# Front of a fused attention and two-MLP kernel: column norms by TensorE, softmax in two halves, split score steps, a new order of the first unit

## What is computed

```
qn = q / (norm(q, axis=tokens) + 1e-6)      # one norm per channel (column)
kn = k / (norm(k, axis=tokens) + 1e-6)
s  = kn.T @ qn / tau                        # 256 x 256
a  = exp(s - max_row(s)); a /= sum_row(a) + 1e-9
x  = v @ a                                  # read as N x 256
x  = gelu(x @ w_in1) @ w_out1               # h * sigmoid(1.702 h)
y  = elu(x @ w_in2) @ w_out2
```

## Time and profile before

| | |
|---|---|
| time, median of 3 runs | 1051.01 us (1050.25 to 1051.07) |
| time of the profiled execution | 1050.98 us |
| its span | 1049.2 us (1.8 us lie around it) |
| PE busy, DVE, ACT, POOL | 98%, 73%, 72%, 1% |
| mean granted PE clock | 0.996 |
| front part, span start to the first `down` product | 72.94 us |

### The profile page before, as it was taken

How to read it: one execution, slowest core, us unless ns; L and a number is a source line. 1 busy time by engine, 2 the same in 40 slices (tenths; PEclk the granted TensorE clock), 3 DMA queues, 4 the chain that set the end, 5 groups by cost and what they waited for, 6 DMA issues and landing times.

```text
span 1049.2 us, 13911 instructions
## 1 busy us (share of the span) xinstructions
PE 1032.1 (98%) x4588; PEld 860.5 (82%) x4588; DVE 763.2 (73%) x1236; ACT 758.0 (72%) x1358; POOL 10.1 (1%) x11
## 2 busy tenths in 40 slices
PE   9999999999999999999998999999999999999996
PEld 7878888888888888888986887887887888888896
DVE  6688756656656655655878788888888888788775
ACT  6586665665666566556778888788788788788884
POOL 0110000000000000000000000000000000000000
PEclk9999999999999999999999999999999999999998
DMA  9913003003003002003122002101201101110112
GB/s 351 285 36 61 1 23 59 1 7 74 1 1 76 3 0 58 1 1 121 41 78 79 1 1 61 21 1 41 40 1 41 33 9 35 22 21 1 21 21 35
DMA packets 106935, 46.24 MB, mean 44 GB/s; under 512 B 90864, under 2 KB 97776, under 8 KB 106224
## 3 DMA queue, kind: packets, MB, share of 16 engines
q1 hardware_dynamic: 106864, 45.36, 16.0%
HBM read 33.03 MB, written 12.32 MB: 43 GB/s over the span
## 4 chain that ended last, share of the span: by engine, by line
PE 91%; ACT 4%; issue 2%; DVE 1%; DMA 0%; DVEq 0%; ACTq 0%; SPq 0%
PE bank L932 29%; PE bank L934 29%; PE bank L933 29%; PE bank L944 4%; ACT xo L599 1%; ACT act_out L537 1%; ACT blk_hi L461 1%; DVE gated L772 1%; PE bank L998 0%; PE bank L999 0%; PE bank L1003 0%; DMA qk<-in_k_dram 0%; ACT g_hi L555 0%; ACT u L497 0%; ACT w_dn_hi L423 0%
## 5 line engine op out<-in xcount | busy, mean ns | idle before, releaser
L932 PE MATMUL bank<-g_hi,w_dn_hi 128*128 128x512 f32 (+1 forms) x768 | 296.3, 386 | 0.7 <-DVE g_lo L785 0.6
L934 PE MATMUL bank<-g_hi,w_dn_lo 128*128 128x512 f32 (+1 forms) x768 | 295.9, 385 | 0.0
L933 PE MATMUL bank<-g_lo,w_dn_hi 128*128 128x512 f32 (+1 forms) x768 | 295.8, 385 | 0.0
L785 DVE TENSOR_TENSOR g_lo<-gated,g_hi 128x512 fp32r<-128x512 f32 (+1 forms) x384 | 259.9, 677 | 48.5 <-ACT g_hi L555 42.4
L932 PE MATMUL bank<-blk_hi,w_up_hi 128*128 128x512 f32 (+1 forms) x672 | 261.5, 389 | 4.1 <-DVE gated L772 1.6
L933 PE MATMUL bank<-blk_lo,w_up_hi 128*128 128x512 f32 (+1 forms) x672 | 259.0, 385 | 0.0
L934 PE MATMUL bank<-blk_hi,w_up_lo 128*128 128x512 f32 (+1 forms) x672 | 259.0, 385 | 0.0
L555 ACT CAST g_hi<-gated 128x512 fp32r<-128x512 f32 (+1 forms) x288 | 175.8, 610 | 21.8 <-DVE gated L772 21.8
L932 PEld LDWEIGHTS bank<-g_hi,w_dn_hi 128*128 128x128 f32 x768 | 144.2, 188 | 28.8 <-DVE g_lo L785 1.8
L933 PEld LDWEIGHTS bank<-g_lo,w_dn_hi 128*128 128x128 f32 x768 | 144.2, 188 | 27.0
L934 PEld LDWEIGHTS bank<-g_hi,w_dn_lo 128*128 128x128 f32 x768 | 144.2, 188 | 27.0
(11 more groups left out here) (110 smaller groups left out, 718.1 us busy)
## 6 DMA issues: line engine op xcount, KB each, us to landing
qk<-in_q_dram SPq DMA_DIRECT2D x14, 384.0 KB, 9.9
qk<-in_k_dram SPq DMA_DIRECT2D x14, 384.0 KB, 10.7
x_scratch<-xo SPq DMA_DIRECT2D x10, 512.0 KB, 3.1
raw<-x_scratch SPq DMA_DIRECT2D x5, 1024.0 KB, 4.8
out_dram<-blocks SPq DMA_DIRECT2D x40, 128.0 KB, 2.7
blocks<-in_v_dram SPq DMA_DIRECT2D x36, 128.0 KB, 3.4
stage<-in_moe_w_in_dram SPq DMA_DIRECT2D x8, 512.0 KB, 5.9
stage<-in_moe_w_out_dram SPq DMA_DIRECT2D x8, 512.0 KB, 5.4
```

The costliest lines, as they stand in the source:

```text
L785: nc.vector.tensor_tensor(g[1][:, x, 0:w], gated[:, n % 2, 0:w], g[0][:, x, 0:w].bitcast(F32), ALU.subtract).then_inc(c_glo, 1)
L932: nc.tensor.matmul(out_ps, w_hi, x_hi, start=start, stop=False, skip_group_check=goes_on)
L933: nc.tensor.matmul(out_ps, w_hi, x_lo, start=False, stop=False, skip_group_check=goes_on)
L934: return nc.tensor.matmul(out_ps, w_lo, x_hi, start=False, stop=stop, skip_group_check=goes_on)
```

## The change

- **Groups.** 20 groups now: 2, 1, 1, 2, twelve of 3, then 2, 1, 1, 1. The first 17 (`LANES`) go through the lanes.
- **Idle turns.** The three dummy matmuls become 14 fp32 matmuls of 128 columns on `ones`, which POOL writes first.
- **Split steps.** In groups 5 to 15 one step each, and groups 17 and 18, is scored by three fp32r passes per half instead of one fp32 matmul. ACT makes the high part (`split_hi`), POOL the low one, DVE for the last two.
- **Norms.** The fold on DVE is gone. The squares of the last three groups go to SBUF, ACT copies the three lanes to SBUF, and PE sums each of these six tiles by four fp32 matmuls with one moving column (`column_sums`), ahead of the last step of group 16. q's and k's norms are then four columns; q's is turned into a row by two fp32 matmuls on the identity (`norm_row`).
- **Halves.** The scores of groups 17 to 19 are done for half 0 first, then for half 1, and the softmax, its transposes and `eT` run by halves between the v transposes.
- **Order.** SP issues v between the parts 1 and 2 of w_in1. ACT splits w_in1 after the norms; the lists of ACT, DVE and PE up to unit 1 are new. The number of `a_w`, product and transpose instructions is the same.

```diff
-    G_STEPS = [3] * 14 + [2, 1, 1, 1]
-    LANES = 15
+    G_STEPS = [2, 1, 1, 2] + [3] * 12 + [2, 1, 1, 1]
+    LANES = NG - 3
+    SPLIT_GROUPS = list(range(5, 16)) + [LANES, LANES + 1]
+    BY_GPSIMD = 11
+    PARTS = 7
+    SQUARES_UP_TO = list(range(1, 15)) + [15, 18, NG, NG, NG, NG]
...
-        aw_ps = banks[4:8]
+        aw_ps = banks[6:8] + banks[4:6]
-        q_sums, k_sums = banks[4][:, 0:C], banks[2][:, 0:KC]
-        eT_ps = banks[2]
+        col_sums, row_ps = banks[4][:, 0:2 * KC], banks[4][:, C:2 * C]
+        eT_ps = [banks[i][:, 0:C] for i in (2, 4)]
...
+        IDLE_TURNS = 14
...
-            for fb in range(FB):
-                load_w_in1(fb)
+            load_w_in1(0)
+            load_w_in1(1)
...
+            load_w_in1(2)
+            load_w_in1(3)
...
+            for i, n in enumerate(SPLIT_GROUPS[:BY_GPSIMD]):
+                pool.wait_ge(c_qkhi, i + 1)
+                nc.gpsimd.tensor_tensor(qk_lo[:, i % PARTS, :, :], qk[:, n % RING, :, 0, :],
+                                        qk_hi[:, i % PARTS, :, :].bitcast(F32), ALU.subtract).then_inc(c_qklo, 1)
...
+            def split_hi(n):
+                i = SPLIT_GROUPS.index(n)
+                act.wait_ge(c_qk[n % RING], 32 * (n // RING + 1))
+                if i >= PARTS:
+                    act.wait_ge(c_score, SPLIT_GROUPS[i - PARTS] + 1)
+                nc.scalar.copy(qk_hi[:, i % PARTS, :, :], qk[:, n % RING, :, 0, :]).then_inc(c_qkhi, 1)
...
+            squared = 0
+                if n == LANES:
+                    act.wait_ge(c_sum, SUM_ZERO + LANES)
+                    nc.scalar.copy(lanes[:, :, :, :], sums[:, :, :, :]).then_inc(c_lanes, 1)
+                if n in SPLIT_GROUPS:
+                    split_hi(n)
+                while squared < SQUARES_UP_TO[n]:
+                    square(squared)
+                    squared += 1
...
+            act.wait_ge(c_norm, 1)
+            nc.scalar.activation(roots, col_sums, ACT.Sqrt).then_inc(c_root, 1)
+            nc.scalar.activation(small[:, 1:2], small[:, 1:2], ACT.Exp)
             w1_hi(0)
-            act.wait_ge(c_norm, 1)
+            w1_hi(1)
...
+            def et_hi(i):
+                act.wait_ge(c_et, i + 1)
+                nc.scalar.copy(eT[0][:, :, i * P:(i + 1) * P], eT_ps[i].rearrange("p (j i) -> p j i", j=KC)).then_inc(c_ethi, 1)
...
+            et_hi(0)
+            w1_hi(2)
+            sum_of_row()
+            et_hi(1)
             nc.scalar.activation(small[:, 1:2], small[:, 1:2], ACT.Gelu_apprx_sigmoid)
+            aw_raw(0)
             block_hi(0, X11)
             block_hi(0, X21)
-            aw_raw(0)
             aw_raw(1)
+            w1_hi(3)
+            up_hi(0, 0)
             block_hi(0, T2)
-            up_hi(0, 0)
             up_hi(0, 1)
-            dn_hi(0)
             block_hi(0, T1)
             aw_raw(2)
+            up_hi(0, 2)
+            copy_u1(0)
+            aw_raw(3)
+            dn_hi(0)
             block_hi(0, T3)
+            up_hi(1, 0)
+            up_hi(1, 1)
+            copy_u2(0)
+            gelu(0, H11)
             block_hi(0, T4)
-            up_hi(0, 2)
-            aw_raw(3)
-            copy_u1(0)
-            up_hi(1, 0)
+            g_hi(0, H11)
+            copy_u3(0)
             aw_raw(4)
             block_hi(0, X22)
-            copy_u2(0)
             aw_raw(5)
-            gelu(0, H11)
-            copy_u3(0)
-            g_hi(0, H11)
             aw_raw(6)
-            up_hi(1, 1)
             gelu(0, H22)
             aw_raw(7)
             g_hi(0, H22)
...
+            dve.wait_ge(c_root, 1)
+            step(nc.vector.tensor_scalar_add(roots, roots, 1e-6))
+            step(nc.vector.reciprocal(inv_q, inv_q))
+            assert steps_done[0] == N_INV_Q
+            step(nc.vector.tensor_scalar(inv_k, inv_k, tau_sb, None, ALU.mult))
+            step(nc.vector.reciprocal(inv_k, inv_k))
-            dve.wait_ge(c_score, NG)
+            dve.wait_ge(c_norm, 2)
+            nc.vector.tensor_copy(rq_row[:], row_ps).then_inc(c_row, 1)
+            dve.wait_ge(c_row, 1)
             for i in range(KC):
+                dve.wait_ge(c_half, i + 1)
...
+            et_lo(0)
+            inverse_of_row()
             copy_v(0)
-            dve.wait_ge(c_rsum, 1)
-            step(nc.vector.reciprocal(inv_sum, row_sum))
-            dve.wait_ge(c_ethi, 1)
-            nc.vector.tensor_tensor(eT[1][:, :, :].rearrange("p j i -> p (j i)"), eT_ps[:],
-                                    eT[0][:, :, :].rearrange("p j i -> p (j i)").bitcast(F32),
-                                    ALU.subtract).then_inc(c_etlo, 1)
+            et_lo(1)
             t_of(0, T1)
             copy_v(1)
             t_of(0, T2)
-            t_of(0, T3)
             block_lo(0, X11)
             block_lo(0, X21)
+            up_sums(0)
+            up_lo(0, 0)
             block_lo(0, T2)
-            up_lo(0, 0)
-            up_sums(0)
-            t_of(0, T4)
-            dn_lo(0, 0)
+            block_lo(0, T1)
+            t_of(0, T3)
             up_lo(0, 1)
-            block_lo(0, T1)
             up_lo(0, 2)
             sum11_of(0)
+            t_of(0, T4)
             block_lo(0, T3)
+            dn_lo(0, 0)
+            up_lo(1, 0)
             up_sums(1)
             block_lo(0, T4)
-            block_lo(0, X22)
             sum22_of(0)
             g_lo(0, H11)
+            block_lo(0, X22)
+            up_lo(1, 1)
             dn_lo(0, 1)
-            up_lo(1, 0)
-            up_lo(1, 1)
...
-            pe.wait_ge(c_zero, 1)
-            for turn in range(3):
-                nc.tensor.matmul(s_ps[turn % KC], scores[:, 0, 0:P], scores[:, 0, :], start=turn < KC, stop=False)
+            pe.wait_ge(c_const, 1)
+            for _ in range(IDLE_TURNS):
+                nc.tensor.matmul(s_ps[0][:, 0:P], ones[:], ones[:], start=True, stop=True)
...
+            def split_step(n, i):
+                part = SPLIT_GROUPS.index(n)
+                if part < BY_GPSIMD:
+                    pe.wait_ge(c_qklo, part + 1)
+                else:
+                    pe.wait_ge(c_qklast, part - BY_GPSIMD + 1)
+                hi, lo, rows = qk_hi[:, part % PARTS, :, :], qk_lo[:, part % PARTS, :, :], slice(i * P, (i + 1) * P)
+                return three_pass(s_ps[i], hi[:, 1, rows], lo[:, 1, rows], hi[:, 0, :], lo[:, 0, :], False, False, True)
+            def column_sums(of, start, stop):
+                for x in range(2 * KC):
+                    mm = nc.tensor.matmul(col_sums[:, x:x + 1], of[:, x // KC, (x % KC) * P:(x % KC + 1) * P], ones[:, 0:1],
+                                          start=start and x == 0, stop=stop, skip_group_check=True)
+                return mm
             def norms():
-                pe.wait_ge(c_fold, GROUP + NG - LANES)
+                for x in range(NG - LANES):
+                    pe.wait_ge(c_sq, LANES + x + 1)
+                    column_sums(sq_last[x], x == 0, False)
+                pe.wait_ge(c_lanes, 1)
+                for lane in range(GROUP):
+                    mm = column_sums(lanes[:, lane, :, :], False, lane == GROUP - 1)
+                mm.then_inc(c_norm, 1)
+            def norm_row():
+                pe.wait_ge(c_dve, N_INV_Q)
+                    mm = nc.tensor.matmul(row_ps[:, i * P:(i + 1) * P], inv_q[:, i:i + 1].to_broadcast([P, P]), ident[:],
...
+            for n in range(LANES):
+                pe.wait_ge(c_qk[n % RING], 32 * (n // RING + 1))
+                split = 1 if n in SPLIT_GROUPS else 0
+                for s in range(split, G_STEPS[n]):
+                    if n == LANES - 1 and s == G_STEPS[n] - 1:
+                        norms()
+                    for i in range(KC):
+                        mm = whole_step(n, s, i)
+                if split:
+                    for i in range(KC):
+                        mm = split_step(n, i)
+                mm.then_inc(c_score, 1)
+            norm_row()
+            for n in range(LANES, NG):
+                pe.wait_ge(c_qk[n % RING], 32 * (n // RING + 1))
+            for i in range(KC):
+                for n in range(LANES, NG):
+                    mm = split_step(n, i) if n in SPLIT_GROUPS else whole_step(n, 0, i)
+                mm.then_inc(c_half, 1)
...
+                if d == 0:
+                    pe.wait_ge(c_vfirst[tile], V_LOAD)
...
+                if n < KC:
+                    pe.wait_ge(c_ethi, i + 1)
+                if n == 2:
+                    pe.wait_ge(c_etlo, KC)
+                if n == 3:
                     pe.wait_ge(c_vcopy, KC)
                 if n >= 4:
+                if n < KC:
+                    pe.wait_ge(c_etlo, i + 1)
...
-            for n in range(5):
-                a_w(n)
+            transpose_first(0)
+            transpose_exp(0)
+            transpose_first(1)
+            transpose_exp(1)
+            transpose_first(2)
+            a_w(0)
+            transpose_first(3)
+            a_w(1)
+            a_w(2)
+            a_w(3)
```

(43 more changed lines are left out.)

113 lines of the change are left out of this document (39 added, 74 removed).

## The result

The changed kernel is slower: median 1056.71 us (1056.41 to 1057.17, 5 runs) against 1051.01 us for the kernel before on the same chip, a ratio of 1.0054 (1.0039 to 1.0069). That is outside the range of the prediction (1047.7 to 1053.0). The profiled execution took 1056.41 us, 5.43 more than that of before.

What follows compares the result with a forecast made beforehand. PE, busy 98% of the span, was taken as the bound, with only its time up to the first `down` product movable. -1.05 - 1.85 + 5.05 - 3.35 = -1.2 us gave 1049.8 us, range 1047.7 to 1053.

Steps and rivals of the forecast that it cites:

- Term 1: The start: turns on `ones` raise PE's clock, so scores start at 6.3 at full clock; -1.05 us, or -1.45.
- rival (d): At the start: the dummies don't raise the clock before the scores do; +1.0 to +1.8 us, 1051; chance 0.1.
- Data is no limit: At the start: three-step groups land every 1.96 to 2.0 us, while PE needs 2.59 for one.
- Term 2: The 13 split steps: 26 fp32 matmuls become 78 passes of 256 columns at 0.12 us; -1.85 us.
- Rival (b): In the split steps: passes of 256 columns wait for their weights; at 0.188 us each, 1055.1; chance 0.08.
- Term 3: The norms: 48 one-column records at 0.112 us and four of `norm_row` added on PE, 0.79 us removed; +5.05 us.
- Rival (a): Behind the norms: the clock falls to half for 3.4 us, moving the end by 1.65; 1051.4; chance 0.2.
- term 4: Softmax to the first `down` product: idle time and slow clock of 4.85 us become 1.5 idle; -3.35 us.

Runs made afterwards that it cites:

- e11: The kernel before with only the 14 turns on `ones` in place of its three dummies, without the memset of `scores`: 1050.18 us, ratio 0.9990 to before.
- e3: The changed kernel with the edits of e1 and e2 together: 1055.46 us, ratio 1.0052 to before.
- e10: e7 with POOL making all 13 low parts, w_in1 loaded and split in another order, two of the last squares in PSUM: 1047.82 us, ratio 0.9963 to before.
- e5: The changed kernel without POOL's 11 split steps, which are scored whole; DVE's two stay split: 1059.26 us, ratio 1.0081 to before.
- e1: The changed kernel with all four high parts of w_in1 made ahead of ACT's root: 1055.07 us, ratio 1.0040 to before.
- e2: The changed kernel with 128 moving columns of `ones` in the norm matmuls in place of one: 1054.01 us, ratio 1.0032 to before.
- e6: e2 with the last low part of w_in1 made by DVE behind `w_up_lo` instead of by POOL: 1051.28 us, ratio 1.0007 to before.
- e7: The changed kernel with last squares and lanes folded on DVE into one tile, 8 one-column records instead of 48: 1050.22 us, ratio 0.9994 to before.
- e8: e7 with w_in1's parts 0 and 1 split ahead of the root, one part later, one last: 1053.28 us, ratio 1.0022 to before.
- e9: e7 with all four parts of w_in1 loaded ahead of v and split ahead of the root: 1052.10 us, ratio 1.0010 to before.

## Why the prediction was wrong, step by step

| step | predicted | in the kernel after |
|---|---|---|
| scores start | 6.3, full clock | 6.02, full clock |
| norms start | 41.9 | 41.68 |
| norms end | 47.3 | 48.13 |
| from there to the first `a_w` | 5.9 | 8.06 |
| first `a_w` to the first `down` | 18.5 | 22.46 |
| first `down` | 71.7 | 78.65 |

**Term 1 was right, its size in part by luck.** The turns bring the clock up ahead of the scores, and rival (d) falls; in e11 the turns alone bring the norms 1.43 us earlier, the better of my two values (1.05 and 1.45). But with the same turns the scores start anywhere from 5.67 to 7.05 in the eleven traces, and my 6.3 is one value out of that. "Data is no limit" holds only just: PE waits for a landing 0.20 us at 11.70 in e3 (scores from 6.04) and 0.37 at 9.71 in e10 (from 5.72).

**Term 2 was right, its price by a small cancelling.** Passes follow at 0.12 as forecast (15.82 to 15.94 to 16.05 in a step); the first pass behind a plain fp32 matmul takes 0.31, but the eight fp32 records behind the step take 1.54 us (16.41 to 17.95) where eight at 0.216 take 1.73, so 0.19 comes back. e5 confirms 0.13 us saved per step. Rival (b), loads that don't overlap, falls. The lower of the two prices that I weighed, from the Trainium skill's "TensorE: Matmul & The Clock Gate", section "Back-to-back issue gap" (262 cycles), isn't what these rows show: 0.12, not 0.109.

**Term 3 was right in the row's price and wrong as a term.** A record costs 0.108 to 0.112, as forecast, while the clock is up. 1.07 us more (6.45 for 5.38) came from the clock's fall within the norms; in e1, where it fell only at their end, the same 48 records take 5.33. (Two small sums are off: term 3 adds up to +5.03, not +5.05, and the idle and slow part of the old stretch to 4.80, not 4.85. Neither matters.)

**Rival (a) came, with a price too small.** I gave it 0.2 and 1.65 us, from the one fall in the trace of before, 3.4 us long. It lasted 6.82 us. In it lie 24 norm records (+1.27 by 3.86 - 2.59), and from 48.13 to 52.49 PE gets 4.36 us of half speed, 2.2 us of work lost; that is the 8.06 - 5.9. Together 3.4 us. The evidence "L954 was only 0.36 us long, so no row tests this" should have weighed for a high chance, not a low one: the one argument against it, that short transposes left the clock up, was about another kind of instruction and 1.2 us of it. The Trainium skill, "TensorE: Matmul & The Clock Gate", "Part 4: PE-mode transpose", says that transposes don't count as busy. No run here tests that. What e2 shows beside the kernel after is that one-column matmuls let the clock fall, and that 128 columns in the same place are enough to keep it.

**Two steps failed.** The first is the full clock that terms 3 and 4 take for granted through the norms and behind them, which I had only as rival (a) at 1.65 us: it cost 1.07 + 2.16 = 3.2. The second, and larger, is the walk of term 4, which lays out DVE's operations with their old durations and so puts what DVE loses beside POOL at nothing. It reads "POOL's low parts of w_in1 come at 5.3, 7.7, 10.0, 13.9 ...: no wait". I used POOL's lateness as POOL's only effect, and I had the sentence "POOL did 1024 columns in 2.34 us with DVE busy beside it" for the converse, which it doesn't hold: it gives POOL's duration, and says nothing about what DVE lost. The old list hid it, because POOL worked from 49.93 to 56.94, where DVE mostly read PSUM. The trace of before did show it once, in a row that I read past. DVE in the kernel before:

```profile
55.93 1.56 DVE L734 TENSOR_TENSOR t_sum<-raw,t_sum 128x512 f32<-128x512 f32 x1
57.42 0.68 DVE L734 TENSOR_TENSOR t_sum<-raw 128x512 f32<-128x512 f32 x1
```

Two operations of one line and size, 1.56 and 0.68, the long one ending 0.55 us behind POOL's 56.94. The new order put the last low part at 61.73, amid DVE's chain to `product1`, and PE stood idle for 2.5 us; with the 1.7 of the second fall of the clock, less 0.24 for the rest, this makes the +3.96 from `a_w` to `down`. e6 takes POOL away from there, and the wait goes from 2.67 to 0.48, so some 2.2 us of it are the meeting. That the second fall comes from the wait is likely, not shown: it came behind waits of 2.35 (the kernel after), 2.33 (e5) and 2.60 (e7), not behind one of 2.67 (e2) or 1.87 (e8), and in e1, e3, e6, e9 and e10, with no wait over 0.5 us ahead of `product1`, it didn't come. The Trainium skill, "GPSIMD Engine Reference", section "8. Key points", states that GpSimd shares its SBUF interfaces with VectorE, with contention for instructions in a two-port mode or with two SBUF inputs. The trace agrees for the two inputs (2.62 beside 0.42). That section gives no price, and the price is what decided. Had I laid it into the walk, the stall would have been in the sum.

The difference is thus, from 71.7: -0.2 (start and splits), +1.07 (norms), +2.16 (half clock behind them), +3.96 = 78.7, against 78.65 in the profile.

**What the range lacked.** Its upper end, 1053, took one price for the clock and none for DVE beside POOL. The rival for "slower" was a matmul that waits for its weights; the true one, a transfer of work to POOL that stops DVE, was not among them.

## What to carry to other kernels

Price a moved instruction twice: by its own duration, and by what its neighbour on the shared memory loses while it runs, and look in the old trace for one operation of the same shape with two durations. Put GpSimd's elementwise work where VectorE reads PSUM. When such work is moved, look for the next operation that it meets: e1, e3, e8 and e9 each traded one meeting for another. Where TensorE has to sum over partitions, fold first, and if many tiles remain let it stream many columns: here 128 cost what one did (0.11 us a record), and 48 narrow records cost the clock for 6.8 us and more.

## What the runs showed of the hardware

- **A DVE operation can stand for as long as POOL's instruction runs.** 2.62 us for 0.42 (after), 4.53 for two of 0.64 (e8), 2.30 and 2.08 for operations on four and two columns with one input (e9; 0.97 and 2.07 in e1, 0.96 and 2.08 in e3), which take 0.17 and 0.23 with POOL idle (the kernel after, from 48.51). With an input in PSUM the time is unchanged (0.42, 0.68, 0.69 in e10), a RECIPROCAL of two columns keeps its 0.17 (e9), and a one-input operation on one column its 0.15 (the kernel after, 53.58). POOL's subtraction, 2.34 in the earlier trace rows as a third of 7.01, loses far less: 2.40 to 2.79.
- **One moving column lets the clock fall, 128 don't.** Same start, same 38 records in 4.00 us, nearly the same DMA load: 0.50 from 45.67 (after), 1.00 throughout (e2). 8 such records do no harm (e7, e10). With 48 such records the fall came 3.0 us after the norms' start in e5, 4.0 in the kernel after, 5.2 in e1. A wait of 2.60 us was followed by a fall in e7, one of 2.67 in e2 wasn't; what decides this is open.
- **128 fp32 columns cost what one costs:** 0.112 us per record over 48 of them (e2), 0.111 with one column at full clock (e1).
- **A switch from plain fp32 to fp32r passes shows 0.31 us for the first pass** and 0.12 for the others (17.95 us in the kernel after, and at each split step); the fp32 matmuls behind it win 0.19 back.
